# Two attention heads beside a gated MLP on TensorE: local and downsampled scores of each pair's second head in one place of the step table

## The chip, the cores and the metric

The kernel runs on one core of one Trainium2 chip. The metric is device time in microseconds (us) of one execution, lower is better. The engines are called TensorE (PE), VectorE (DVE), ScalarE (ACT), GpSimd (POOL) and SyncE (SP, which issues the DMAs).

## What is computed

Three stages in a row, all in float32. First attention over q, k, v of shape (4, 8, 576, 64), in two forms that are added:

```python
q_d = q.reshape(B, H, Sd, factor, D).mean(axis=3)     # factor = 4, Sd = 144; k_d, v_d alike
out_up = np.repeat(sm_attn(q_d, k_d, v_d), factor, axis=2)
mask = np.abs(pos[:, None] - pos[None, :]) < factor
attn = softmax(np.where(mask, scale * q @ k.T, -1e9))
x = out_up + attn @ v                                 # then (B * S, H * D) = (2304, 512)
```

Then an MLP `h = x @ w_in; x = (h * cos(h)) @ w_out` with 2048 hidden units, and a second one, gated, behind an RMS norm, with 1536 hidden units: `silu(xn @ w_gate) * (xn @ w_val) @ w_out`.

## The kernel before, in words

**Tiles.** The 2304 tokens are six chunks of 384. The four batches of attention are 576 tokens each, and a batch is four pairs of heads (`PAIRS`), a head taking 64 of the 128 partitions. Each dense product is made of three matmuls (L1274 to L1276), of high and low parts that ScalarE, VectorE and GpSimd split off.

**A chunk of the first MLP** (`chunk1`) is a loop over 16 + 3 steps. In step f TensorE does `up`, the hidden block f (12 matmuls of 384 columns, shown as `xs,W`), and then `down` of hidden block f - 3 (9 matmuls of 512 columns, shown as `W,ring`). Beside it the hidden block f goes through ScalarE and VectorE: turns (L751), VectorE's L1053 and L1055, the absolute value (L757), the sine (L759), the product on VectorE (L1061), the high part on ScalarE (L686, `g_high`, one step later) and the low part on VectorE (L972). `up(f)` needs the product of f - 3, `down(f)` the low part of f.

**Attention beside it.** Batch 0 is done ahead of the chunks (`Wide`). Batches 1 to 3 are done in chunks 0 to 2 (`Narrow`, loops with `Fori(0, ACH)`), pair after pair, cut into steps. Where a step stands is written out by hand, in tables of (step f, half): half 0 is between `up` and `down` on TensorE, half 1 behind `down`; on ScalarE half 0 is behind turns and `g_high`, before the absolute value, half 1 behind the sine; on VectorE half 0 is behind L1055 and half 1 behind L1061. `PE_WHERE` (L350) has the places of TensorE's six steps, `BESIDE_WHERE` (L357) those of ScalarE and VectorE; a row is a pair, `steps_at` reads them, the three functions `attend` issue what stands at a place. The steps are:

- `scores0`, `local1`, `downsampled1` on TensorE: `local` (L1187 to L1193) lays down a mask with three bf16 matmuls and adds ten products of 64x64 windows; `downsampled` (L1210) is two products over 144 downsampled positions. Both heads of a pair use the same PSUM bank for the local scores (`X`), and another one for the downsampled scores (`Z`), also for the transposes and values.
- `less_max0` and `exps` on VectorE: `less_local_max` (L905 to L912) subtracts the row maximum, `down_max` (L918, L920) makes the bias of the downsampled exponential, `sum_up` (L931 to L938) the reciprocal of the sum. In `exps` VectorE does less_local_max of head 1, sum_up of head 0, down_max of head 1, sum_up of head 1.
- `exps` on ScalarE: the exponential of the downsampled scores (L626) and of the local ones (L617) of head 0, then local and downsampled of head 1, with a table load in front (and one before the next sine).
- GpSimd multiplies by the reciprocals (`normalise`, L507 and L510); then `transposes0`, `transposes1` (L1227, L1230) on TensorE, each followed by two copies (`copy_pt0/1`: L643 on ScalarE, L943 on VectorE), then `values` (L1243, L1251), `copy_down` (L652), and the additions into XY (`add_up`, L893).

**Waits that the edit meets.** All orders are fixed, and an engine that waits holds up all that it has behind. Local scores of head 1 wait until VectorE has taken up those of head 0:

```python
pe.wait_ge(diff_ready, u)          # local, s == 1
pe.wait_ge(exp_down, u)            # downsampled, s == 1: ScalarE has taken up head 0's
pe.wait_ge(exp_down, u + 2)        # transposes, s == 0
pe.wait_ge(x_ready, n)             # local, s == 0: the additions of the pair before
```

`values` waits for both heads' copies. SyncE loads the next Q and K (`load_qk`) when the downsampled scores of the pair are done.

Of the kernel before, what the change touches and what calls it, by code (L numbers as in the profile page):

```python
# [81 lines left out]
def attention_and_two_mlps(nc, qk, vwin, vgrp, w1, wgv, w2, rms_g, const, wsplit, out):  # L82
# [256 lines left out]
    def hold(eng, semaphore, value):  # L339
# [3 lines left out]
        if not isinstance(value, int):  # L343
# [3 lines left out]


    PE_STEPS = ("scores0", "local1", "downsampled1", "transposes0", "transposes1", "values")
    PE_WHERE = (((1, 0), (2, 0), (3, 0), (4, 0), (4, 1), (5, 0)),  # L350
# [3 lines left out]


    BESIDE_STEPS = ("down_qk", "less_max0", "exps", "copy_pt0", "copy_pt1", "copy_down")
    BESIDE_WHERE = (((-1, 1), (0, 0), (1, 1), (2, 1), (3, 1), (4, 1)),  # L357
# [3 lines left out]

    def steps_at(names, where, place):
        return [(name, j) for j in range(PAIRS) for name, at_ in zip(names, where[j]) if at_ == place]
# [247 lines left out]
    def act_program(act):  # L611
# [76 lines left out]
        def attend(c, f, half):  # L688

            for what, j in steps_at(BESIDE_STEPS, BESIDE_WHERE, (f, half)):  # L690
                if what == "exps":
# [175 lines left out]
    def dve_program(dve):  # L867
# [106 lines left out]
        def attend(c, f, half):  # L974

            for what, j in steps_at(BESIDE_STEPS, BESIDE_WHERE, (f, half)):
                if what == "down_qk":
# [191 lines left out]
    def pe_program(pe):  # L1169
# [127 lines left out]
        def attend(b, step, half):  # L1297

            for what, j in steps_at(PE_STEPS, PE_WHERE, (step, half)):
                if what == "scores0":  # L1300
# [210 lines left out]
```

## Time and profile before

| what | value |
|---|---|
| median of three runs | 998.36 us (997.68 to 998.68) |
| profiled execution | 998.75 us; span of its instructions 996.6 us |
| PE busy | 960.0 us, 96% of the span, 6104 matmuls |
| PE weight loads | 852.7 us, 86% |
| DVE busy | 576.2 us, 58% |
| ACT busy | 502.7 us, 50% |
| POOL busy | 313.9 us, 32% |
| mean granted clock | 0.993 of full |
| the three chunks with attention | about 56 to 356 us |

The busy figures are shares of the whole span. PE is the engine with little rest. A matmul's length in the timeline is longer than the distance from its start to the next one's, as they overlap: distances of starts tell what one costs. A timeline row with x20 or x4 is a run of matmuls counted as one, with the two passes of a float32 product counted apart. Idle time of an engine stands in brackets at the end of a row, with what ended it.

### The profile page before, as it was taken

To read this page: it belongs to the slowest core of one execution; us is meant where nothing else is said; L and a number is where in the kernel's file an instruction comes from. 1 tells how busy PE (TensorE), PEld (TensorE's weight loads), DVE (VectorE), ACT (ScalarE), POOL (GpSimd) and SP (SyncE) were. 2 spreads that over 40 slices of the span, in tenths; PEclk is the share of its full clock that TensorE was granted. 3 is DMA by queue.
4 is the path that set the end of the run, shared out by engine and by line. 5 is a ranking of instruction groups with operands and counts; after the bars stand their busy time and mean duration, and the time that the engine had idled before them with its cause. 6 is when DMAs were issued, how large, how long until landed. Compare 5 with 4: busy or idle time off the path is not lost.

```text
span 996.6 us, 17754 instructions
## 1 busy us (share of the span) xinstructions
PE 960.0 (96%) x6104; PEld 852.7 (86%) x6104; DVE 576.2 (58%) x1225; ACT 502.7 (50%) x1081; POOL 313.9 (32%) x366
## 2 busy tenths in 40 slices
PE   7899998999899999999999899999999999999998
PEld 6677787888788889899988788899899999999997
DVE  6767766766676665564557544455744445544434
ACT  4456665666566667676666533333522224423322
POOL 5937862321232146568486112111300001000000
PEclk9999999999999999999999899999999999999999
DMA  9522110211021025434344575555565455575531
GB/s 305 192 95 93 54 52 25 80 55 52 26 80 53 22 76 185 164 147 169 126 170 149 210 253 149 154 152 161 149 217 151 149 161 166 153 229 158 160 106 64
DMA packets 66176, 132.35 MB, mean 133 GB/s; under 512 B 7088, under 2 KB 7216, under 8 KB 66096
## 3 DMA queue, kind: packets, MB, share of 16 engines
q1 hardware_dynamic: 66096, 131.27, 41.4%
q8 instruction: 52, 0.85, 0.4%
q14 instruction: 28, 0.23, 0.1%
HBM read 104.50 MB, written 26.74 MB: 132 GB/s over the span
## 4 chain that ended last, share of the span: by engine, by line
PE 75%; DVE 9%; ACT 7%; issue 4%; POOL 4%; DMA 1%; DVEq 0%; ACTq 0%; POOLq 0%; SPq 0%
PE ps L1274 23%; PE ps L1276 23%; PE ps L1275 23%; DVE ub L1055 2%; DVE ub L1053 2%; ACT ub L757 2%; PE ps L1193 2%; POOL W L521 2%; PE ps L1210 1%; ACT ub L759 1%; PE ps L1350 1%; DVE XY L893 1%; ACT ub L751 1%; DVE ub L1061 1%; ACT probd L626 1%
## 5 line engine op out<-in xcount | busy, mean ns | idle before, releaser
L1274 PE MATMUL ps<-xo,wu 128*128 128x384 f32 x504 | 169.5, 336 | 5.2 <-ACT gate_a L806 3.7
L1275 PE MATMUL ps<-xo,wu 128*128 128x384 f32 x504 | 170.5, 338 | 0.0
L1276 PE MATMUL ps<-xo,wu 128*128 128x384 f32 x504 | 170.0, 337 | 0.0
L1274 PE MATMUL ps<-xs,W 128*128 128x384 f32 x384 | 136.0, 354 | 0.9 <-DVE xs L968 0.9
L1276 PE MATMUL ps<-xs,W 128*128 128x384 f32 x384 | 131.7, 343 | 4.8 <-issue 4.8
L1275 PE MATMUL ps<-xs,W 128*128 128x384 f32 x384 | 131.3, 342 | 0.0
L1274 PE MATMUL ps<-W,ring 128*128 128x512 f32 x288 | 116.5, 405 | 0.0
L1276 PE MATMUL ps<-W,ring 128*128 128x512 f32 x288 | 113.5, 394 | 0.0
L1275 PE MATMUL ps<-W,ring 128*128 128x512 f32 x288 | 113.4, 394 | 0.0
L1274 PEld LDWEIGHTS ps<-xo,wu 128*128 128x128 f32 x504 | 95.3, 189 | 12.4 <-ACT gate_a L806 4.1
L1275 PEld LDWEIGHTS ps<-xo,wu 128*128 128x128 f32 x504 | 95.1, 189 | 6.7
L1061 DVE TENSOR_TENSOR ub<-ub,ps 128x384 f32<-128x384 f32 x96 | 53.0, 552 | 73.6 <-ACT ub L759 73.6
L1276 PEld LDWEIGHTS ps<-xo,wu 128*128 128x128 f32 x504 | 95.2, 189 | 0.0
L757 ACT ACTIVATE ub<-ub 128x384 f32<-128x384 f32 x96 | 50.4, 525 | 72.1 <-DVE ub L1055 72.1
L1276 PE MATMUL ps<-wo,ring 128*128 128x512 f32 x216 | 85.7, 397 | 0.0
L1275 PE MATMUL ps<-wo,ring 128*128 128x512 f32 x216 | 85.4, 395 | 0.0
L1274 PE MATMUL ps<-wo,ring 128*128 128x512 f32 x216 | 85.3, 395 | 0.1
L1274 PEld LDWEIGHTS ps<-xs,W 128*128 128x128 f32 x384 | 74.0, 193 | 12.2 <-issue 7.7
L1101 DVE TENSOR_TENSOR val_b<-val_b,ps 128x384 f32<-128x384 f32 x36 | 19.9, 554 | 100.7 <-ACT val_b L806 100.5
L1275 PEld LDWEIGHTS ps<-xs,W 128*128 128x128 f32 x384 | 74.1, 193 | 1.8
L1053 DVE TENSOR_SCALAR ub<-ub 128x384 f32<-128x384 f32 x96 | 46.8, 488 | 49.1 <-ACT ub L751 49.0
L1276 PEld LDWEIGHTS ps<-xs,W 128*128 128x128 f32 x384 | 73.9, 192 | 0.0
(134 smaller groups left out, 1852.3 us busy)
## 6 DMA issues: line engine op xcount, KB each, us to landing
wu<-wsplit SPq DMA_DIRECT2D x252, 256.0 KB, 2.8
wsplit<-wp SPq DMA_DIRECT2D x84, 256.0 KB, 2.0
W_raw<-w SPq DMA_DIRECT2D x8, 1024.0 KB, 15.1
qk<-qk SPq DMA_DIRECT2D x14, 576.0 KB, 4.0
gv<-wgv SPq DMA_DIRECT2D x12, 512.0 KB, 3.6
vw<-vwin SPq DMA_DIRECT2D x14, 384.0 KB, 3.2
out<-XY SPq DMA_DIRECT2D x18, 256.0 KB, 3.4
vg<-vgrp SPq DMA_DIRECT2D x26, 144.0 KB
```

The source lines that it names most:

```text
L521: g.tensor_tensor(lo, raw, hi.bitcast(F32), ALU.subtract).then_inc(unit_ready, 1)
L626: ins = a.activation(kind.probd[j][0:QT, s, t, :], kind.sd[s][:, t * SD:t * SD + SD], ACT.Exp, scale=SCALE_D, bias=dbias[0:QT, s, t:t + 1] ...
L751: a.activation(v, HB[f % NH], ACT.Identity, scale=INV_2PI, bias=consts[:, 0:1]).then_inc(turns_ready, 1)
L757: a.activation(v, v, ACT.Abs).then_inc(abs_ready, 1)
L1053: v.tensor_scalar(w, w, MAGIC, -2.0 * math.pi, ALU.subtract, ALU.mult).then_inc(angle0, 1)
L1055: v.tensor_tensor(w, w, HB[f % NH], ALU.add).then_inc(angle_ready, 1)
L1061: v.tensor_tensor(w, w, HB[f % NH], ALU.mult).then_inc(g_done, 1)
L1101: v.tensor_tensor(vb[:, :], vb[:, :], CB, ALU.add).then_inc(vb_ready, 1)
L1193: ins = t_.matmul(sl[64 * half:64 * half + 64, t * WIN:t * WIN + WIN], q[:, Q0[w]:Q0[w] + WIN], k[:, K0[w]:K0[w] + WIN], start=False, stop ...
L1274: t_.matmul(dst, a_lo, b_hi, start=first, stop=False, skip_group_check=True)
L1275: t_.matmul(dst, a_hi, b_lo, start=False, stop=False, skip_group_check=True)
L1276: return t_.matmul(dst, a_hi, b_hi, start=False, stop=last, skip_group_check=True)
```

## The change

The places of `local1` and `downsampled1` become one place in each row of `PE_WHERE`. For pairs 0 and 1 it is half 1 of the step in which `local1` stood (steps 2 and 6), for pairs 2 and 3 the place of `downsampled1` (steps 10 and 14). `exps` of pairs 0 and 1 move from half 1 of a step to half 0 of the next. Chunks without attention, batch 0 and the second MLP have no such table.

```diff
--- before.py
+++ after.py
@@ -347,15 +347,15 @@
 
 
     PE_STEPS = ("scores0", "local1", "downsampled1", "transposes0", "transposes1", "values")
-    PE_WHERE = (((1, 0), (2, 0), (3, 0), (4, 0), (4, 1), (5, 0)),
-                ((5, 1), (6, 0), (6, 1), (7, 1), (8, 0), (8, 1)),
-                ((9, 0), (9, 1), (10, 0), (11, 1), (12, 0), (12, 1)),
-                ((13, 0), (13, 1), (14, 0), (15, 0), (16, 0), (16, 1)))
+    PE_WHERE = (((1, 0), (2, 1), (2, 1), (4, 0), (4, 1), (5, 0)),
+                ((5, 1), (6, 1), (6, 1), (7, 1), (8, 0), (8, 1)),
+                ((9, 0), (10, 0), (10, 0), (11, 1), (12, 0), (12, 1)),
+                ((13, 0), (14, 0), (14, 0), (15, 0), (16, 0), (16, 1)))
 
 
     BESIDE_STEPS = ("down_qk", "less_max0", "exps", "copy_pt0", "copy_pt1", "copy_down")
-    BESIDE_WHERE = (((-1, 1), (0, 0), (1, 1), (2, 1), (3, 1), (4, 1)),
-                    ((4, 0), (5, 1), (5, 1), (6, 1), (7, 1), (8, 1)),
+    BESIDE_WHERE = (((-1, 1), (0, 0), (2, 0), (2, 1), (3, 1), (4, 1)),
+                    ((4, 0), (5, 1), (6, 0), (6, 1), (7, 1), (8, 1)),
                     ((8, 0), (9, 0), (9, 1), (11, 0), (12, 0), (12, 1)),
                     ((12, 0), (13, 0), (13, 1), (14, 1), (15, 1), (16, 1)))
```

TensorE, chunk 0 to 2, pair 0, steps 2 and 3; the difference, with `qk_77` the loaded Q and K, `qkd_83` the downsampled ones, `xs,W_49` the operands of an up block:

```order
 L1193 MATMUL ps<-qk_77 64x64 x10
+L1210 MATMUL ps<-qkd_83 72x144 x2
 L1320 REGISTER_ALU
 L1274 MATMUL ps<-xs,W_49 128x384
...
 L1276 MATMUL ps<-xs,W_49 128x384
-L1210 MATMUL ps<-qkd_83 72x144 x2
 L1327 REGISTER_ALU
```

The downsampled scores of head 1 are moved from behind the up block of step 3 to a place ahead of it, right behind the local scores.

ScalarE, pair 0, steps 1 and 2, before:

```order
L759 ACTIVATE ub<-ub,consts 128x384
L621 ISA
L626 ACT_TABLE_LOAD
L626 ACTIVATE probd_82,sums<-ps,dbias 72x144 x2
L617 ACTIVATE prob_81<-prob_81 128x320
L615 REGISTER_ALU
L617 ACTIVATE prob_81<-prob_81 128x320
L626 ACTIVATE probd_82,sums<-ps,dbias 72x144 x2
L748 REGISTER_ALU
L751 ACTIVATE ub<-ps,consts 128x384
L681 REGISTER_ALU
L686 ACTIVATE ring<-ub 128x384
```

and now:

```order
L759 ACTIVATE ub<-ub,consts 128x384
L748 REGISTER_ALU
L751 ACTIVATE ub<-ps,consts 128x384
L681 REGISTER_ALU
L686 ACTIVATE ring<-ub 128x384
L621 ISA
L626 ACT_TABLE_LOAD
L626 ACTIVATE probd_82,sums<-ps,dbias 72x144 x2
L617 ACTIVATE prob_81<-prob_81 128x320
L615 REGISTER_ALU
L617 ACTIVATE prob_81<-prob_81 128x320
L626 ACTIVATE probd_82,sums<-ps,dbias 72x144 x2
```

Turns of step 2 and the high part of step 1 have gone ahead of the four exponentials.

TensorE, pair 3, steps 13 and 14; `W_50,ring` is a down block, `xs,W_51` an up block:

```order
 L1276 MATMUL ps<-W_50,ring 128x512
+L1320 REGISTER_ALU
+L1274 MATMUL ps<-xs,W_51 128x384
...
 L1181 ISA
 L1187 MATMUL ps<-maskb,identb 128x64
...
 L1193 MATMUL ps<-qk_77 64x64 x10
-L1320 REGISTER_ALU
-L1274 MATMUL ps<-xs,W_51 128x384
...
 L1210 MATMUL ps<-qkd_83 72x144 x2
```

The up block of step 14, 12 matmuls, has moved from behind the local scores of head 1 to a place ahead of them; pair 2 is alike.

## Rows read from the trace of the kernel before

**Rows 1.** TensorE's waits in the whole run: who waited for whom, total, times, longest
```profile
PE ps L1276 <- issue: 4.8, 2, 2.6
PE ps L1187 <- DVE XY L893: 4.6, 6, 1.5
...
PE ps L1210 <- ACT probd L626: 1.2, 3, 0.7
PE ps L1227 <- DVE probd L943: 1.2, 3, 0.4
```

**Rows 2.** Timeline of TensorE, chunk 0, pair 1: start us, length us, engine, line, operation [idle before]
```profile
93.28 0.39 PE L1275 MATMUL ps<-W,ring 128*128 128x512 f32 x1
93.51 0.39 PE L1276 MATMUL ps<-W,ring 128*128 128x512 f32 x1
93.83 0.71 PE L1210 MATMUL ps<-qkd 64*72 64x144 f32 x4
94.47 0.44 PE L1274 MATMUL ps<-xs,W 128*128 128x384 f32 x1
94.75 0.34 PE L1275 MATMUL ps<-xs,W 128*128 128x384 f32 x1
94.92 0.34 PE L1276 MATMUL ps<-xs,W 128*128 128x384 f32 x1
```

**Rows 3.** Timeline of TensorE, chunk 0, pair 0
```profile
66.42 0.20 PE L1187 MATMUL ps<-maskb,identb 128*128 128x64 bf16 x1
...
67.39 0.44 PE L1274 MATMUL ps<-xs,W 128*128 128x384 f32 x1
...
69.42 0.34 PE L1276 MATMUL ps<-xs,W 128*128 128x384 f32 x1
70.00 0.71 PE L1210 MATMUL ps<-qkd 64*72 64x144 f32 x4 [0.24 <-ACT probd L626]
70.63 0.50 PE L1274 MATMUL ps<-W,ring 128*128 128x512 f32 x1
```

**Rows 4.** Timeline of TensorE: waits behind pair 0, chunks 0 and 1
```profile
78.15 0.52 PE L1227 MATMUL ps<-ident,prob 128*128 128x128 f32 x3 [0.38 <-DVE probd L943]
...
86.42 0.20 PE L1187 MATMUL ps<-maskb,identb 128*128 128x64 bf16 x1 [1.46 <-DVE XY L893]
...
188.06 0.20 PE L1187 MATMUL ps<-maskb,identb 128*128 128x64 bf16 x1 [0.45 <-DVE XY L893]
```

**Rows 5.** Timeline of ScalarE, chunk 0, pairs 0 and 1
```profile
67.82 1.28 ACT L626 ACT_TABLE_LOAD   x1
...
96.12 0.57 ACT L751 ACTIVATE ub<-ps,consts 128x384 f32<-128x384 f32 x1
96.59 0.52 ACT L686 ACTIVATE ring<-ub 128x384 fp32r<-128x384 f32 x1
97.71 0.52 ACT L757 ACTIVATE ub<-ub 128x384 f32<-128x384 f32 x1 [0.60 <-DVE ub L1055]
```

**Rows 6.** Timeline of VectorE, chunk 0, pair 0
```profile
67.83 0.56 DVE L1061 TENSOR_TENSOR ub<-ub,ps 128x384 f32<-128x384 f32 x1 [0.77 <-ACT ub L759]
...
70.33 0.49 DVE L931 TENSOR_REDUCE sums<-prob 128x5 f32<-128x320 f32 x1 [1.01 <-ACT prob L617]
...
71.27 0.40 DVE L918 TENSOR_REDUCE dmax<-ps 72x2 f32<-72x288 f32 x1
```

**Rows 7.** Stretches of 2 us in and at the end of chunk 0: PE busy, granted clock, DMA
```profile
86.00:88.00 2.00, 1.58 (x27) 1.00 0.00 0
157.00:159.00 2.00, 0.00 (x0) 1.00 0.00 0
159.00:161.00 2.00, 1.70 (x9) 0.94 0.01 4
161.00:163.00 2.00, 2.00 (x8) 0.50 0.04 8
163.00:165.00 2.00, 2.00 (x13) 0.71 0.00 0
```

**Rows 8.** Timeline of VectorE, chunk 1, pair 3
```profile
237.96 0.49 DVE L905 TENSOR_REDUCE lmax<-ps 128x5 f32<-128x320 f32 x1 [0.70 <-PE ps L1193]
...
238.90 0.47 DVE L931 TENSOR_REDUCE sums<-prob 128x5 f32<-128x320 f32 x1
...
240.90 0.45 DVE L918 TENSOR_REDUCE dmax<-ps 72x2 f32<-72x288 f32 x1 [0.99 <-PE ps L1210]
...
250.02 0.45 DVE L943 COPY probd<-ps 72x288 f32<-72x288 f32 x1
```

**Rows 9.** Timeline of TensorE, chunk 1, pair 3
```profile
250.57 0.71 PE L1243 MATMUL ps<-probd,vd 72*64 72x144 f32 x8
```

## The prediction

> **What bounds the kernel now.** I read the waits first. Over the run TensorE waits for other engines in few places, and inside the three attention chunks for three things: the next pair's local scores wait six times for the additions into XY, 4.6 us; the second head's downsampled scores wait three times for the exponentials of the first head, 1.2 us; the second head's transposes wait three times for a copy, 1.2 us [rows 1]. So TensorE is the bound. An edit is worth the time it takes off TensorE's own stream, less each wait it adds there, and a new wait is refilled only where an old one stood behind it.
>
> Then the timelines of TensorE. A downsampled cluster between two dense blocks runs from the start of the last down matmul at 93.51 to the second up matmul at 94.75: 1.24 us. Two regular steps would take 0.23 and 0.17 us [rows 2], so the cluster costs 0.84 us, of which 0.64 us is its own (93.83 to 94.47) and 0.20 us the way in and out. In the page's tables this looks like a busy engine, so the 0.20 us is seen only between starts.
>
> Last the order of ScalarE and VectorE beside it. The exponential of the downsampled scores of head 0 must be done before TensorE overwrites the same bank with head 1's. In pair 0 TensorE already arrives 0.24 us early for it, with a whole up block (67.39 to about 69.6) between local and downsampled scores [rows 3]. That block is the cover of the exponential.
>
> **The change, part by part.**
>
> *Switching saved.* One way in and out less for each pair, four pairs in three chunks: 12 x 0.20 = 2.4 us at most. The Trainium skill, page "TensorEngine Tiling (Array Packing)", section "Tiling Modes", has it that going from one tiling mode to another drains the engine; the trace agrees, at 0.20 us a time, and by that rule alone the kernel would come to 998.4 - 2.4 = 996.0 us.
>
> *Pair 0.* Local 1 stays where it is (step 2 has no down block), and downsampled 1 moves ahead of the up block of step 3. At the same time the exponentials of pair 0 move behind turns and the high-part copy of the hidden block on ScalarE. Today the table load starts at 67.82 [rows 5] and the cluster at 70.00 [rows 3]: 2.18 us from the one to the other. After the change ScalarE does L751 at 67.82, then L686, which is issued 0.47 us after it (96.12 to 96.59) [rows 5] and also needs the product that VectorE ends at 67.83 + 0.56 = 68.39 [rows 6]. L686 then runs from 68.4 to 68.96, and the cluster can start at 68.96 + 2.18 = 71.1. TensorE is done with local 1 at about 67.5, so it stands still for 3.6 us. The up block, formerly cover, now comes after the cluster: the down block starts 1.1 us (the exponential is later) plus 2.2 us (an up block: 67.39 to 69.42 and one step) later, 3.3 us in all. VectorE's and ScalarE's own work there is moved by about the 1.1 us only, and it no longer has turns and angle to do behind it, so what is late next is TensorE itself.
> Old waits behind it take some back: 0.4 us before the transposes [rows 4], and before the next pair's scores 0.4 us in chunks 1 and 2 and up to 1.5 us in chunk 0 [rows 1, 4]. Chunk 0 has the longer one because VectorE and GpSimd are slow there, and that chain moves too (the transposes feed it), so I take 1.1 of the 1.5. Left: 1.8, 2.5 and 2.5 us, 6.8 us.
>
> *The clock behind this wait.* At the end of chunk 0 TensorE stands still for 2.6 us. The granted clock then falls to 0.50, that is from 2.4 to 1.2 GHz: 0.94 over one stretch of 2 us, 0.50 over the next, 0.71 over the third [rows 1, 7]. This adds up to 2 x (0.06 + 0.50 + 0.29) / 0.5 = 3.4 us at half clock, 1.7 us of work lost. The wait of 1.5 us in chunk 0 was followed by full clock, 1.00 from 86 to 88 us [rows 4, 7]. The new wait of 3.6 us lies beyond 2.6, so I take the loss three times. Without it the sum is 4.7 us smaller.
> The Trainium skill, page "TensorE: Matmul & The Clock Gate", section "Why this matters for your kernels", warns of idle gaps between bursts of matmuls in the middle of a kernel, which is a rule against this change; by it the three gaps cost three slow stretches, without it the total would be 1006.7 instead of 1011.4 us.
> With the loss, chunk 0 has TensorE so late that its whole old wait is filled: 3.3 + 1.7 - 0.4 - 1.5 = 3.1; chunks 1 and 2: 3.3 + 1.7 - 0.4 - 0.4 = 4.2. Together 11.5 us (6.8 without it).
>
> *Pair 1.* Scores of head 1 stand after the down block of step 6, and the exponentials one half-step later, behind L751 and L686 of step 6. These two leave the path behind the exponentials (96.12 to the L757 at 97.71, 1.6 us [rows 5]), while local 1 is a down block later and with it the chain of sums, +1.1 us (worked out under pair 3). So the two side engines come out 0.5 us earlier, and TensorE's wait before pair 2's scores shrinks; TensorE gains 0.20 us of switching and pays 0.1 to 0.3 us at the new cluster, since the exponential ends just after local 1: behind the up block ScalarE needs about 0.4 (to take it up) + 0.5 + 0.5 (L751, L686 [rows 5]) + 2.2 = 3.6 us, TensorE 9 x 0.23 = 2.1 for the down block [rows 2], 0.2 to turn and 1.0 for local 1 (66.42 to 67.39 [rows 3]), 3.3 us. I take 0.4 us gained per chunk (bounds 0.1 and 0.65): -1.2 us.
>
> *Pair 2.* Local 1 moves behind an up block, exponentials stay. Side engines come 1.1 us later, but the transposes wait at (11, 1) and (12, 0), where the trace has room. Only the switching: 3 x 0.2 = -0.6 us.
>
> *Pair 3.* The same move, but with the transposes at (15, 0) and (16, 0) there is no room. VectorE starts on local 1 at 237.96; behind an up block (2.13 us) it starts at 240.09. Then less_local_max takes 0.94 us (237.96 to 238.90 [rows 8]) and sum_up 0.94 us (70.33 to 71.27 [rows 6]), so the maximum of the downsampled scores starts at 241.97 instead of 240.90 [rows 8], 1.07 us later. All behind it shifts: the last copy starts at 251.1 instead of 250.02 [rows 8] and ends 0.45 us later, 251.55; the values product needs it and started at 250.57 [rows 9], 0.10 us after it. It now starts at 251.65, 1.1 us later, though TensorE has saved 0.2 us. Nothing in the rest of the chunk waits that could take it back. Bounds: -0.2 us (if a margin hides it) to +1.3; taken +1.1, three times: +3.3 us.
>
> DMAs, register work and table loads stay the same in number, SyncE and GpSimd keep their order; GpSimd's normalising and the queue of Q, K loads (which wait for the downsampled scores) move by the same few tenths and have whole steps of room, so they cost nothing; if that cover were gone, a load, 4.0 us to landing in the page's table of DMA issues, would show before L1187.
>
> **Sum:** 11.5 - 1.2 - 0.6 + 3.3 = +13.0 us. The profiled execution took 998.75 us (span 996.6, some 2.2 around it), so its like becomes 1011.8; against the median of 998.36, 0.4 us lower, I predict **1011.4 us**.
>
> **The rivals.**
> *The clock holds.* Whether 3.6 us of rest costs the clock each time is read from one place only, and where it falls late, part of the slow stretch passes in the wait. All three kept: +8.3 us, 1006.7 us; one kept, 1009.8. Chance 0.20 for two or three kept.
> *Chunk ends absorb it.* TensorE stops for 2.6 us at the end of a chunk for nothing that the trace names. If that is a wait with a fixed end, two such places could give back up to 4.8 us: 1006.6 us. Against: it comes with the loop's jump, after TensorE's own last block. Chance 0.08.
> *Faster.* If the downsampled exponentials of pairs 0 and 1 were done by the end of local 1, the 12 ways in and out would be all that is left, and pair 0's old 0.24 us waits would go too: 998.4 - 2.4 - 0.7 = 995.3 us. It decides at 67.5 us in chunk 0: the exponential must be ready there, and today it is ready at 70.0. Chance 0.03.
> *Nothing moves.* The delays all vanish in later waits: 998 us. There are only 1.7 us of waits per chunk behind them. Chance 0.02.
> *Worse.* Slow stretches twice as long, as a longer rest may bring: +5.1, 1016.5 us. Chance 0.05.
>
> **How the numbers follow.** The forecast keeps 0.62. Its own bounds (pair 1, pair 3, one clock loss) reach from 1008 to 1013.5. Taking in the held clock and part of pair 3's lower bound, the range is 1004.5 to 1014.5. About 0.2% (2 us) is what a measurement of this kernel can tell from no change. Slower by more: 0.95; within: 0.02; faster: 0.03.
>
> **What would show it.** In the new profile: a wait of L1210 for L626, three times 3.5 us or so; the granted clock at 0.5 for some 3.4 us behind each; the waits of L1227 for L943 in pair 0 gone and new ones in pair 3, with L1243 behind them; L1187's wait for L893 down from 4.6 to under 2.5 us. Wrong would be: L1210's wait under 1.5 us in total, the clock at 1.00 in the attention chunks, or chunks 0 to 2 longer by less than 2 us each.

## The result, and the profile after

The changed kernel takes 1012.42 us (median of six executions, 1008.96 to 1017.41), the kernel before 998.34 us beside it. The ratio is 1.0152 with a 95% interval of 1.0119 to 1.0184: 1.5% slower, within the range forecast and 1 us from the predicted 1011.4 us. The profiled execution is the slowest of the six, 1017.41 us with a span of 1015.3 us, 18.7 us more than the span before. It is some 5 us above the median. Part of that is the clock (a mean of 0.983, where the six executions have 0.983 to 0.990); 1.1 us of the growth lies ahead of the chunks, where TensorE comes to chunk 0's first mask at 63.69 us instead of 62.61. The clock alone doesn't order these six: 1014.01 us also has 0.983, and 1016.54 us has 0.985.

TensorE's waits over the whole run, which answer to [rows 1] (who waited for whom, total, times, longest):

```profile
PE ps L1210 <- ACT probd L626: 12.3, 6, 4.2
...
PE ps L1276 <- issue: 4.9, 2, 2.6
PE ps L1227 <- DVE probd L943: 4.7, 5, 1.3
...
PE ps L1187 <- DVE XY L893: 2.8, 2, 1.5
```

The downsampled scores' wait has gone from 1.2 to 12.3 us, that for the copy from 1.2 to 4.7 (1.3 of it lies ahead of the chunks), and the old wait for the additions into XY fell from 4.6 to 2.8. The net of these three is 12.8 us, 11.5 without the 1.3 ahead of the chunks.

The timeline of TensorE in chunk 0, pair 0, answers to [rows 3]:

```profile
67.50 0.20 PE L1187 MATMUL ps<-maskb,identb 128*128 128x64 bf16 x1
...
67.74 0.80 PE L1193 MATMUL ps<-qk 64*64 64x64 f32 x20
72.22 1.23 PE L1210 MATMUL ps<-qkd 64*72 64x144 f32 x4 [3.68 <-ACT probd L626]
73.38 0.69 PE L1274 MATMUL ps<-xs,W 128*128 128x384 f32 x1
```

and that of ScalarE beside it to [rows 5]:

```profile
68.79 0.56 ACT L751 ACTIVATE ub<-ps,consts 128x384 f32<-128x384 f32 x1
69.50 0.52 ACT L686 ACTIVATE ring<-ub 128x384 fp32r<-128x384 f32 x1 [0.15 <-DVE ub L1061]
70.04 1.28 ACT L626 ACT_TABLE_LOAD   x1
```

From the mask of local 1 to the downsampled cluster TensorE takes 4.72 us (67.50 to 72.22); 71.14 - 66.42 = 4.72 us was worked out. The table load starts 0.54 us after L686, and the cluster 2.18 us after that. The cluster then takes 1.16 us (72.22 to 73.38) where it took 0.63 before (70.00 to 70.63): the clock is at half (0.50 from 72 to 74 us). The stretches of chunk 0 (length, PE busy, granted clock, DMA), which answer to [rows 7]:

```profile
68.00:70.00 2.00, 0.54 (x20) 1.00 0.00 0
70.00:72.00 2.00, 0.00 (x0) 0.52 0.00 0
72.00:74.00 2.00, 1.78 (x6) 0.50 0.00 0
74.00:76.00 2.00, 2.00 (x8) 0.50 0.71 200
76.00:78.00 2.00, 2.00 (x9) 0.77 0.44 168
92.00:94.00 2.00, 1.73 (x28) 0.99 0.59 146
94.00:96.00 2.00, 2.00 (x7) 0.50 1.00 280
96.00:98.00 2.00, 2.00 (x9) 0.65 0.89 342
```

The clock falls to 1.2 GHz during the wait of 3.7 us and stays there for 2 x (0.48 + 0.50 + 0.50 + 0.23) / 0.5 = 6.8 us, twice as long as forecast; some 2.1 us of it pass in the wait, before 72.22. It falls once more at 94 us, and there only a wait of 1.54 us lies ahead (L1187 at 92.27). The kernel before had a wait of 1.46 us at that place and kept full clock [rows 4, 7]. The same stretches in chunks 1 and 2, where the clusters start at 183.50 and 288.32 us:

```profile
182.00:184.00 2.00, 0.50 (x2) 0.68 0.00 0
184.00:186.00 2.00, 2.00 (x8) 0.50 0.10 12
186.00:188.00 2.00, 2.00 (x7) 0.50 0.89 286
188.00:190.00 2.00, 2.00 (x7) 0.61 0.19 71
288.00:290.00 2.00, 1.68 (x6) 0.63 0.00 0
290.00:292.00 2.00, 2.00 (x7) 0.51 0.62 164
```

They add up to 6.8 and 3.4 us at half clock.

The periods from one pair's first mask (L1187) to the next pair's, or for pair 3 to the next chunk's first, before -> after, us:

| chunk | pair 0 | pair 1 | pair 2 | pair 3 and chunk end |
|---|---|---|---|---|
| 0 | 23.81 -> 28.58 | 23.11 -> 24.23 | 23.26 -> 24.97 | 31.94 -> 33.03 |
| 1 | 23.33 -> 27.95 | 21.77 -> 21.41 | 23.25 -> 23.11 | 31.53 -> 32.83 |
| 2 | 22.83 -> 26.31 | 21.77 -> 21.40 | 23.24 -> 23.12 | as far as the next up block: 23.19 -> 24.45 |

Chunk 1's pair 3, the timeline of TensorE and then of VectorE, which answer to [rows 9] and [rows 8]:

```profile
258.76 0.49 PE L1227 MATMUL ps<-ident,prob 128*128 128x128 f32 x3
...
262.72 0.52 PE L1227 MATMUL ps<-ident,prob 128*128 128x128 f32 x3 [1.11 <-DVE probd L943]
...
265.72 0.71 PE L1243 MATMUL ps<-probd,vd 72*64 72x144 f32 x8
```

```profile
253.95 0.49 DVE L905 TENSOR_REDUCE lmax<-ps 128x5 f32<-128x320 f32 x1 [2.81 <-PE ps L1193]
...
255.82 0.40 DVE L918 TENSOR_REDUCE dmax<-ps 72x2 f32<-72x288 f32 x1
...
262.13 0.45 DVE L943 COPY probd<-ps 72x288 f32<-72x288 f32 x1
...
265.17 0.45 DVE L943 COPY probd<-ps 72x288 f32<-72x288 f32 x1
```

The second transposes of the pair (262.72) now stand 1.11 us for VectorE's copy of the first, and the values start 0.10 us behind the next one, as before.

### The profile page after: what moved, and what is told of

Same layout as the page of the kernel before. It is cut to its first block, busy times and chain, and to the rows that moved or that the text cites. A ratio compares the mean times of both kernels' runs of the same rounds, so it can differ in the third digit from the quotient of the medians.

```text
span 1015.3 us, 17754 instructions
## 1 busy us (share of the span) xinstructions
PE 966.8 (95%) x6104; PEld 861.3 (85%) x6104; DVE 574.2 (57%) x1225; ACT 502.8 (50%) x1081; POOL 313.2 (31%) x366
## 4 chain that ended last, share of the span: by engine, by line
PE 77%; DVE 8%; ACT 6%; issue 4%; POOL 4%; DMA 1%; SPq 0%; DVEq 0%; ACTq 0%; POOLq 0%
PE ps L1274 24%; PE ps L1276 23%; PE ps L1275 23%; POOL W L521 1%; DVE ub L1053 1%; PE ps L1193 1%; DVE ub L1055 1%; PE ps L1210 1%; ACT ub L757 1%; ACT ub L759 1%; PE ps L1350 1%; PE ps L1251 1%; PE ps L1227 1%; DVE ub L1061 1%; ACT ub L751 1%
## 5 line engine op out<-in xcount | busy, mean ns | idle before, releaser
L1276 PE MATMUL ps<-xo,wu 128*128 128x384 f32 x504 | 169.8, 337 | 0.0
L1274 PE MATMUL ps<-xs,W 128*128 128x384 f32 x384 | 138.5, 361 | 0.9 <-DVE xs L968 0.9
L1276 PE MATMUL ps<-xs,W 128*128 128x384 f32 x384 | 134.3, 350 | 4.9 <-issue 4.9
L1275 PE MATMUL ps<-xs,W 128*128 128x384 f32 x384 | 133.8, 348 | 0.0
L1276 PE MATMUL ps<-W,ring 128*128 128x512 f32 x288 | 114.0, 396 | 0.0
L1276 PEld LDWEIGHTS ps<-xo,wu 128*128 128x128 f32 x504 | 95.0, 188 | 0.0
L1274 PEld LDWEIGHTS ps<-xs,W 128*128 128x128 f32 x384 | 76.1, 198 | 13.0 <-issue 8.8
L1276 PE MATMUL ps<-wo,ring 128*128 128x512 f32 x216 | 85.7, 397 | 0.0
L1275 PEld LDWEIGHTS ps<-xs,W 128*128 128x128 f32 x384 | 76.5, 199 | 2.0
L1276 PEld LDWEIGHTS ps<-xs,W 128*128 128x128 f32 x384 | 75.9, 198 | 0.0
```

The source lines that it names most:

```text
L1274: t_.matmul(dst, a_lo, b_hi, start=first, stop=False, skip_group_check=True)
L1275: t_.matmul(dst, a_hi, b_lo, start=False, stop=False, skip_group_check=True)
L1276: return t_.matmul(dst, a_hi, b_hi, start=False, stop=last, skip_group_check=True)
```

## The experiments

Ratios are to the kernel before, run on the same chip.

**Pair 0 undone.** The change, with the old row of pair 0:

```diff
-    PE_WHERE = (((1, 0), (2, 1), (2, 1), (4, 0), (4, 1), (5, 0)),
+    PE_WHERE = (((1, 0), (2, 0), (3, 0), (4, 0), (4, 1), (5, 0)),
-    BESIDE_WHERE = (((-1, 1), (0, 0), (2, 0), (2, 1), (3, 1), (4, 1)),
+    BESIDE_WHERE = (((-1, 1), (0, 0), (1, 1), (2, 1), (3, 1), (4, 1)),
```

> The change with pair 0's row (and its exponentials) as before; pairs 1, 2 and 3 stay changed. Theory A (pair 0's uncovered exponential and the clock behind it cost most): 998.3 - 1.2 - 0.6 + 3.3 = 999.8 us, L1210's wait for L626 down to about 1.5 us in total, granted clock at half only at the chunk ends. Rival B (the cost is spread over the clusters, about 14.1 us over four pairs): 998.3 + 10.6 = 1008.9 us.

Measured: 1001.31 us, 1.0045 [1.0027, 1.0062], which is 4.5 us over the kernel before where 1.5 was forecast and 10.6 by the rival. L1210's wait is down to 1.7 us in total, and no half clock shows between the chunk ends in its profile. So pair 0 carries about 10.7 of the 15.2 us (1.52% less 0.45%). What is left of the other three pairs is larger than the sum had it; its interval, 2.7 to 6.2 us, leaves out the 1.5.

**Pair 0 alone.** The reverse edit, on the kernel before.

> The kernel before with pair 0's row and exponentials changed, pairs 1 to 3 as before. Theory A: 998.3 + 11.5 = 1009.8 us (6.8 us of it the wait and the lost cover, 4.7 the clock), waits of 3.7 us at L1210 three times. Rival B: 998.3 + 3.5 = 1001.8 us.

Measured: 1009.74 us, 1.0122 [1.0105, 1.0139], +12.2 us, where 11.5 was forecast. Its waits in the profile:

```profile
PE ps L1210 <- ACT probd L626: 11.6, 3, 4.2
```

Three waits of 3.9 us on average. Rival B is out from both sides.

**Pairs 1 and 2 alone.** Both rows changed, with pair 1's exponentials, pairs 0 and 3 as before.

> The kernel before with pairs 1 and 2 changed only. Theory A: one way in and out of the tiled products saved six times and a shorter wait for XY: 998.3 - 1.8 = 996.5 us. Rival B: 998.3 + 7 = 1005 us.

Measured: 995.61 us, 0.9991 [0.9975, 1.0006], that is 0.9 us less with an interval from 2.5 less to 0.6 more. Rival B's 1005 us is excluded; 1.8 us of gain lies inside the interval, and so does none. So where its exponential is covered, the cluster costs nothing that the time shows. The waits at L1210 in pair 1 are the forecast 0.25 us.

**Pair 3 alone.** Its row changed, all else as before.

> The kernel before with pair 3's row changed only. Theory A: local 1 behind an up block makes the second transposes and the values wait for VectorE's copy, 1.1 us in each of three chunks: +3.3 us over the kernel before, ratio 1.0033; waits of L1227 for L943 of 1.1 us three times more. Rival D: the cluster only saves the way in and out and the wait is hidden: -0.6 us, ratio 0.9994.

Measured: 1000.80 us, 1.0043 [1.0026, 1.0059], +4.3 us, with an interval from 2.6 to 5.9 that holds the forecast 3.3. The waits:

```profile
PE ps L1227 <- DVE probd L943: 4.5, 6, 1.1
```

This holds the three old waits and three new ones of 1.1 us. Rival D is out. This pair accounts for what is left once pair 0 is undone (4.3 of 4.5 us). The three parts run by themselves add up to 12.2 - 0.9 + 4.3 = 15.6 us, the change by its ratio to 15.2.

**Exponentials of pair 0 back in their place.** The change with `(1, 1)` instead of `(2, 0)` in `BESIDE_WHERE`, row 0.

> The change, with pair 0's exponentials back in half 1 of step 1, TensorE's cluster as changed. Theory A: the exponential is ready 1.1 us earlier, L1210 waits 2.5 us instead of 3.7 us three times, so 3.4 us less than the change, 1009.0 us, if the clock still falls behind it, and up to 5 us less again where it does not. Rival E (the early place was what held ScalarE and VectorE up, and the move is what helps): no gain over the change, 1012.4 us or more.

Measured: 1007.03 us, 1.0103 [1.0078, 1.0128], 4.9 us less than the change by ratio, though the two intervals touch (the change has 1.0119 to 1.0184), so the trace is the firmer evidence. The pair's wait:

```profile
70.94 0.71 PE L1210 MATMUL ps<-qkd 64*72 64x144 f32 x4 [2.54 <-ACT probd L626]
```

2.54 us as forecast. So of the two moves in pair 0, that of the cluster ahead of its cover costs 2.5 us of wait and that of the exponentials another 1.1. The gain beyond 3.4 us fits a clock that falls less often (0.986 to 0.992 over its executions, 0.983 to 0.990 for the change): in its profile chunk 0 keeps 1.00 behind the 2.54 us, chunks 1 and 2 have 3.4 us at half clock each. The interval is too wide to say so from the time alone.

**Exponentials of pair 1 left in their place.** Pairs 1 and 2 alone, with `(5, 1)` for `exps` of pair 1.

> Pairs 1 and 2 changed, with pair 1's exponentials left in half 1 of step 5. Theory A: L1210's waits of 0.25 us in pair 1 go, but ScalarE and VectorE wait for local 1 with turns of step 6 behind them, so the additions into XY come about 1.6 us later: L1187's wait for L893 grows by about 1 us a chunk, and the kernel takes about 3 us more than with the exponentials moved: 998.5 us, ratio 1.001 or 1.002 to the kernel before. Rival F (only TensorE's own waits count): 0.7 us less than with them moved, ratio 0.998.

Measured: 998.82 us, 1.0016 [0.9999, 1.0033], 2.5 us more by ratio than with them moved, on another chip; the two intervals overlap (the other reaches 1.0006), so the time alone does not prove a cost. The ratio is the one theory A gave, the place is not: L1187's wait for L893 stays at 4.6 us, and the waits for the copy grow:

```profile
PE ps L1227 <- DVE probd L943: 6.8, 10, 1.7
PE ps L1276 <- issue: 5.2, 2, 2.6
PE ps L1187 <- DVE XY L893: 4.6, 6, 1.5
PE ps L1210 <- ACT probd L626: 1.0, 3, 0.5
```

Of the 6.8 us 2.1 lie ahead of the chunks; pair 1's second transposes wait 1.07, 1.10 and 1.11 us, where with the exponentials moved they do not wait. The delay of ScalarE and VectorE shows one step earlier than I had it, at the second transposes, just as in pair 3. The half-step that the change gave pair 1's exponentials keeps these waits away.

**The wait filled.** The change, with products that do no work of the kernel between the two steps of pair 0; b counts batches, and bank 4 is free then:

```diff
                     local(Narrow, b, j, 1)
+                    if j == 0:
+                        pe.wait_ge(y_copied, TT * b)
+                        for _ in range(60):
+                            t_.matmul(ps[:, 4, 0:P], identb[:, :], identb[:, :], start=True, stop=True)
```

> The change, with 60 bf16 products of 128x128 by 128 columns added between local and downsampled scores of pair 0's second head, into a bank that nobody reads then; they do no work of the kernel. They should run for about 3.4 us of the 3.7 us of wait. Theory A with the clock (rest of TensorE costs clock): the wait falls to about 0.3 us, the clock stays at 1.00 behind it, and the kernel gets faster by 4 to 6 us, 1007 us, although TensorE has more to do. Rival C (only the wait costs, the clock would not matter or falls anyway): 1012.4 us or slightly more.

Measured: 1008.00 us, 1.0116 [1.0100, 1.0133]. Its interval and the change's overlap, so both were run again beside each other on one chip:

> The change itself once more, on the same chip as the two runs that follow. Ratio to the kernel before 1.0152 [1.0119, 1.0184] as measured; the mean granted clock lower in slower executions, since what differs between executions of one kernel is how often a rest of TensorE costs the clock.

> The change with the 60 products that fill pair 0's wait, beside the change on the same chip. Theory A with the clock: 3.5 to 5 us less than the change, ratio to it 0.9955. Rival C: no difference. Every execution should have a higher mean clock than those of the change, 0.992 to 0.996 against 0.983 to 0.990.

Measured: the change 1013.86 us, 1.0150 [1.0124, 1.0177]; filled 1005.13 us, 1.0076 [1.0053, 1.0098]. With 60 products more in each of three chunks the kernel is 7.4 us faster by the ratios. In the filled kernel's timeline and stretches:

```profile
65.44 0.20 PE L1187 MATMUL ps<-maskb,identb 128*128 128x64 bf16 x1
...
66.41 3.52 PE L1307 MATMUL ps<-identb 128*128 128x128 bf16 x60
70.16 0.71 PE L1210 MATMUL ps<-qkd 64*72 64x144 f32 x4 [0.23 <-ACT probd L626]
```

```profile
68.00:70.00 2.00, 1.94 (x35) 1.00 0.03 8
70.00:72.00 2.00, 1.84 (x11) 1.00 0.16 16
72.00:74.00 2.00, 2.00 (x12) 1.00 0.83 293
74.00:76.00 2.00, 2.00 (x12) 1.00 0.18 60
```

The distance from mask to cluster is the change's 4.72 us (65.44 to 70.16), so the exponential is no earlier; only the clock differs. Rival C is out. What is not settled is the exact size: the same filled kernel gave 1.0116 the first time and 1.0076 the second, on the same chip, and these two intervals do not meet. The first time four of six executions had a mean clock of 0.992 (1007.9 to 1009.6 us), the second time one of six (1008.41 us): at the same clock the same time, so the two differ in how often the clock fell.

The executions of the two kernels on that chip, time in us and mean granted clock:

```
the change   1020.90 0.980   1013.64 0.985   1009.14 0.990   1013.86 0.985   1014.66 0.985
filled       1004.95 0.993   1003.37 0.995   1005.31 0.993   1008.41 0.992   1004.61 0.995   1005.30 0.993
```

Here a slower execution is one with a lower mean clock, within a kernel and between the two.

**The end of a chunk.** Whether the stop of 2.6 us there could take up delays was a rival. TensorE's two chunk loops are written out, first with pairs 1 and 2 changed, then on the kernel before with nothing else:

```diff
-        with pe.Fori(0, ACH) as c:
+        for c in range(ACH):
             chunk1(c, True)
-        with pe.Fori(ACH, LASTC) as c:
+        for c in range(ACH, LASTC):
             chunk1(c, False)
```

> Pairs 1 and 2 changed, and TensorE's loops over chunks 0 to 4 written out as straight code instead of a loop of the machine. The stop of 2.6 us at a chunk's end, which the trace gives to no engine, and the half clock behind it (1.7 us). Theory G (it belongs to the jump back of the loop): both vanish at the two ends between chunks 0 and 2, 996.0 - 4.9 - 3.4 = 988 us. Rival H (it is a wait with a fixed end that the trace does not name, so that the end of a chunk could absorb delays): the stops stay, 996 us.

> The kernel before with TensorE's chunk loops written out and nothing else. If the gain of the version with pairs 1 and 2 changed and the loops written out (0.9943) comes from the loop's end: 997 - 4.9 us = 992 us, ratio 0.995, or down to 0.992 where the half clock behind the stop goes too; L1276's wait at the chunk ends gone. If it came from the pairs alone: 0.999.

Measured: 992.28 us, 0.9943 [0.9926, 0.9960], and 992.71 us, 0.9944 [0.9924, 0.9964]. The waits of the second in its attention chunks:

```profile
PE ps L1187 <- DVE XY L893: 3.8, 5, 1.4
PE ps L1210 <- ACT probd L626: 3.6, 3, 1.7
```

The stop for "issue" at L1276 (an idle time for which the profile names no other engine) is gone from both, so it belongs to the jump back of TensorE's own loop and has no fixed end. The change's own profile says the same: its chunks are longer, and the two stops are still 2.56 and 2.29 us, where they were 2.57 and 2.26. A delay in a chunk is carried through. The second loop, over chunks 3 and 4, jumps back once and shows no wait of TensorE in the profile before, so it is not every jump that costs. The gain is 5.7 and 5.6 us, and not the 8.3 us forecast for the loops in the first: TensorE arrives earlier at pair 0's exponential, where in the second its wait grows from 1.2 to 3.6 us in total. The changed pairs 1 and 2 add nothing that can be measured. Both versions are faster than both kernels, by an edit that has nothing to do with the change.

## Why the prediction was right, point by point

The parts come out on the forecast's side and in its places, but each a little dearer: 12.2 us for pair 0 (11.5 forecast), -0.9 for pairs 1 and 2 (-1.8), +4.3 for pair 3 (+3.3). That the median lies only 1 us from the forecast is in part luck, since executions of the change spread over 8.5 us, in the main by how often the clock falls.

*Pair 0's wait.* Right: 3.6 us forecast, 3.68, 4.15 and 3.68 us in the profile; taking the row away or adding it alone moves the time by 10.7 and 12.2 us, where 11.5 was forecast with the clock. The 4.15 us in chunk 1 answers to the 0.73 us that this chunk waited before, where the others waited 0.24:

```profile
172.62 0.71 PE L1210 MATMUL ps<-qkd 64*72 64x144 f32 x4 [0.73 <-ACT probd L626]
```

*The clock.* The mechanism was right, the size was not. I took one stretch of 3.4 us at half clock behind each of the three waits, 5.1 us of work lost, 4.7 after what an old wait gives back. In the profiled execution there are stretches of 6.8, 6.8 and 3.4 us, of which some 2.1 and 0.8 us pass in the first two waits. Work loses half of the rest: my estimate from these rows is 2.3 + 3.0 + 1.7 = 7.0 us. Two more stretches of 3.4 us stand in chunk 0 behind waits of 1.54 and 1.22 us, another 3.4 us lost, which the sum did not have at all. Pair 0's periods grew by 4.8, 4.6 and 3.5 us instead of 3.1, 4.2 and 4.2; pairs 1 and 2 of chunk 0, forecast at -0.4 and -0.2, grew by 1.1 and 1.7 us from those two. By the filled kernel the clock of pair 0's wait is worth 7.4 us beside the change run again, 3.6 us by the first pair of ratios; so the term of 4.7 is the one that was mis-sized in the profiled execution, and over many it is not known better than this. That the wait of 1.5 us in the kernel before kept full clock was read from one execution, and taken as a rule of the place. My rival "worse", with stretches twice as long, came partly true: of nine waits of 3.68 to 4.26 us in three profiles, six had 6.8 us and three had 3.4 us at half clock. Part of such a stretch passes in the wait itself, so its price in this execution was 7.0 - 5.1 = 1.9 us and not the 5.1 I gave. The Trainium skill, page "TensorE: Matmul & The Clock Gate", section "Why this matters for your kernels", warns of idle gaps between bursts of matmuls; the filled wait agrees with it, at 7.4 us.

*Pair 1.* Right in chunks 1 and 2: -0.36 and -0.37 us against -0.4, with the 0.25 us at the cluster within the 0.1 to 0.3 given.

*Pair 2.* -0.14 and -0.12 us against -0.2: the period gains less than the 0.20 us between starts. The Trainium skill's rule that a change of tiling mode drains the engine (page "TensorEngine Tiling (Array Packing)", section "Tiling Modes") agrees in sign, at 0.12 to 0.14 us a time. The grouped steps still differ in their tiles (64*64 and 64*72 in the timeline), so a change between them may remain; no run separates it. In chunk 0 its second transposes wait 0.19 us.

*Pair 3.* Right: the maximum starts 1.87 us behind the row maximum of local 1 (253.95 to 255.82), 1.88 worked out; the wait is 1.08, 1.11 and 1.11 us in chunks 0 to 2, and the periods grew by 1.09, 1.30 and 1.26 us against 1.1. The row alone gives +4.3 us for a forecast of 3.3, and what the further 1.0 us is stays open, inside the interval. Pair 0's waits for the copy are gone, as forecast.

*Old waits that give back.* L1187's wait fell to 2.8 us, forecast under 2.5. In chunk 0 it did not vanish (1.54 and 1.22 us are left): VectorE's chain there moves with the transposes (from the second transposes to the next mask 8.27 us before, 8.21 after), so the 1.5 us that I let the late TensorE fill in full were not given back. This is the step of pair 0's sum that failed. In chunks 1 and 2 they are gone.

*The rivals.* That the chunk end absorbs delays was wrong, as the loops written out show. "Faster" fails at its own point: the exponential came 3.7 us after local 1. Its price was also short: pair 0's old waits are 0.24, 0.73 and 0.24 us, 1.2 and not 0.7.

## What to carry to other kernels

To put two steps next to each other saves a switch, here 0.12 to 0.20 us a time (too little to show in the time of a run), but what stood between them was the cover of a wait: look up when the second step's input is ready, and move the pair only where another block stays in front (pair 1) and where nothing behind it lives from the earlier result (pair 3 did). A wait on TensorE of the sizes in the table below is to be priced with the clock behind it, and the price read from several executions, since one may have kept it by luck. Where a wait can't be avoided, matmuls put into it that do no work of the kernel can pay: here they made the whole 3.6 to 7.4 us faster.

## What the runs showed that I had not expected

Rests of 1.2 to 1.5 us cost the clock in some executions and not in others: the profiled execution of the kernel before kept 1.00 behind 1.46 us, that of the change fell to 0.50 behind 1.54 and 1.22. All waits of TensorE of 1 us and more in the chunks with attention, from the thirteen profiles of all kernels here, with the cases where a stretch at half clock began in the wait or within 2.5 us behind it:

| wait, us | for what | seen | with half clock |
|---|---|---|---|
| 1.07 to 1.12 | the copy (L1227) | 24 | 0 |
| 1.15 to 1.57 | the additions into XY (L1187), chunk 0 | 26 | 12 |
| 1.65 to 1.71 | the exponential (L1210), loops written out | 4 | 3 |
| 1.82 to 2.64 | the end of a chunk (L1276) | 22 | 16 |
| 2.54 | the exponential, its place of before | 3 | 2 |
| 3.68 to 4.26 | the exponential, as changed | 9 | 9 |

Of the 26 in the second row, the six in the three kernels' profiles that have pair 0's full wait ahead of them all lost the clock, the other twenty only six times. Whether the earlier loss makes the later one likelier was not tested. This makes a kernel with more such rests not only slower but more spread: 1009.1 to 1020.9 us in five executions for the change on one chip, 1003.4 to 1008.4 us in six with the largest rest filled.

TensorE's first chunk loop, the one with attention, stops for 1.8 to 2.6 us where it jumps back, and the clock mostly falls with it (0.94, 0.50, 0.71 in [rows 7]; 16 times of 22 in the table). Written out, the loops save 5.6 of 998 us.
